# The odd rows of the first output chunk, stored by nine of the sixteen DMA engines over SP's and GpSimd's queues

## The reference, cut to what matters

```python
def _attn_ref(q, k, v, g_norm):                    # (8, 8, 576, 64) each
    kv = np.einsum('bhsd,bhse->bhde', k, v)
    out = np.einsum('bhsd,bhde->bhse', q, kv)
    rms = np.sqrt(np.mean(out * out, axis=-1, keepdims=True) + 1e-06)
    return out / rms * g_norm

def _moe_ref(x, phi, w1, w2):                      # x (4608, 512), phi (512, 32), 8 experts, 1024 hidden
    logits = x @ phi
    d = exp(logits - logits.max(0)); d /= d.sum(0) + 1e-09
    slot_input = (d.T @ x).reshape(8, 4, 512)
    for e in range(8):
        slot_out[e] = np.maximum(slot_input[e] @ w1[e], 0.0) @ w2[e]
    c = exp(logits - logits.max(1)); c /= c.sum(1) + 1e-09
    return c @ slot_out.reshape(32, 512)           # (4608, 512), float32
```

## Time and profile before

| | before |
|---|---|
| median of 3 runs | 172.56 us |
| the profiled execution's own time | 172.53 us |
| its span, first to last instruction | 171.2 us |
| mean share of time in which the 16 DMA engines were busy | 98.2% (three kinds of queue together) |
| moved | 71.67 MB, 419 GB/s over the span |
| PE / DVE / ACT / POOL busy | 149.1 / 86.0 / 88.9 / 57.2 us |
| issue of the four stores, SP | 144.24, 151.57, 157.04, 161.19 us |
| last store, issue to landing | 9.9 us |

### The profile page before, as it was taken

The page is one execution under the profiler, slowest core; times in us unless marked ns, Lnnn a source line. Parts: engine busy times, 40 slices in busy tenths (PEclk is TensorE's granted clock), DMA queues, the critical chain, the costliest instruction groups (busy, mean ns, idle before and its releaser), DMA issues.

```text
span 171.2 us, 4497 instructions
## 1 busy us (share of the span) xinstructions
PE 149.1 (87%) x1975; PEld 108.1 (63%) x1975; DVE 86.0 (50%) x184; ACT 88.9 (52%) x230; POOL 57.2 (33%) x68
## 2 busy tenths in 40 slices
PE   7787897989999899999899999999999988989400
PEld 3467776979688888898797775455565444445100
DVE  1122156283677265763936798724897027137400
ACT  2037576786965887768849864203213025137400
POOL 6000708548356755466482579200000000000000
PEclk9999999999999999999999999999999999999965
DMA  5999999999999999999999999998999999999995
GB/s 192 416 422 433 439 415 437 472 421 474 417 413 458 430 426 430 406 404 452 433 492 419 431 429 389 434 450 354 436 478 387 461 390 421 439 396 439 406 459 241
DMA packets 3476, 71.67 MB, mean 419 GB/s; under 512 B 384, under 2 KB 384, under 8 KB 384
## 3 DMA queue, kind: packets, MB, share of 16 engines
q1 hardware_dynamic: 3456, 71.38, 97.6%
HBM read 61.94 MB, written 9.44 MB: 417 GB/s over the span
## 4 chain that ended last, share of the span: by engine, by line
PE 47%; DMA 26%; ACT 12%; DVE 5%; SPq 2%; issue 1%
PE psum L204 47%; DMA arena<-in_kv_dram 13%; DMA arena<-in_w_dram 13%; ACT bd L204 3%; ACT sq L204 3%; ACT xall L204 2%; SPq L204 2%; DVE logits L204 1%; ACT arena L204 1%; DVE ms L204 1%; ACT part L204 1%; ACT d L204 1%; ACT r L204 1%; DVE r L204 0%; DVE d L204 0%
## 5 line engine op out<-in xcount | busy, mean ns | idle before, releaser
L204 PE MATMUL psum<-bd,arena 128*128 128x192 f32 (+1 forms) x320 | 56.1, 335 | 1.9 <-ACT bd L204 1.5
L204 PEld LDWEIGHTS psum<-bd,arena 128*128 128x128 f32 (+1 forms) x320 | 45.4, 179 | 7.1 <-ACT bd L204 2.8
L204 DVE TENSOR_REDUCE ms<-sq 128x16 f32<-128x1024 f32 (+1 forms) x19 | 22.1, 1162 | 32.6 <-ACT sq L204 32.3
L204 POOL TENSOR_TENSOR xall<-xall,r 128x512 f32<-128x512 f32 x34 | 34.8, 1044 | 0.0
L204 POOL TENSOR_TENSOR part<-part,r 128x512 f32<-128x512 f32 x17 | 17.8, 1049 | 49.7 <-DVE r L204 49.7
L204 ACT ACTIVATE sq<-psum 128x512 f32<-128x512 f32 x36 | 21.5, 598 | 12.6 <-PE psum L204 12.4
L204 PE MATMUL psum<-arena 128*64 128x64 f32 (+1 forms) x640 | 21.7, 226 | 3.3 <-DMA arena<-in_kv_dram 2.2
L204 PEld LDWEIGHTS psum<-arena 128*64 128x64 f32 (+1 forms) x640 | 19.0, 137 | 7.9 <-DMA arena<-in_kv_dram 3.5
L204 ACT COPY xall<-psum 128x512 f32<-128x512 f32 x34 | 20.6, 606 | 0.0
L204 ACT COPY part<-psum 128x256 f32<-128x256 f32 (+1 forms) x38 | 13.6, 359 | 9.9 <-DVE part L204 8.8
L204 DVE TENSOR_REDUCE logits<-part 128x64 f32<-128x512 f32 (+1 forms) x18 | 17.8, 991 | 0.0
(11 more groups left out here) (74 smaller groups left out, 118.9 us busy)
## 6 DMA issues: line engine op xcount, KB each, us to landing
arena<-in_w_dram SPq DMA_DIRECT2D x4, 4096.0 KB, 19.9
arena<-in_w_dram SPq DMA_DIRECT2D x1, 7168.0 KB, 27.5
arena<-in_t_dram SPq DMA_DIRECT2D x1, 6912.0 KB, 36.1
arena<-in_w_dram SPq DMA_DIRECT2D x1, 5120.0 KB, 17.9
arena<-in_kv_dram SPq DMA_DIRECT2D x2, 2304.0 KB, 23.4
arena<-in_kv_dram SPq DMA_DIRECT2D x1, 4608.0 KB, 42.6
out_dram<-arena SPq DMA_DIRECT2D x2, 2304.0 KB, 9.6
arena<-in_kv_dram SPq DMA_DIRECT2D x1, 3584.0 KB, 32.2
```

Source lines behind the costliest of these rows:

```text
L204: inst = getattr(engine, method)(*args, **kwargs)
```

## The change

The first store (chunks 0 to 2, 128 rows of 18432 bytes) is taken apart. The odd rows of chunk 0 (64 rows of 6144 bytes) are stored by themselves as soon as chunk 0 is there, in four transfers (`APART`): GpSimd's queue (POOL) stores 21 of them in a transfer whose outer dimension has 3 steps, and then 11 of them, each cut in two, with an outer dimension of 2; SP's queue stores 30 with an outer dimension of 5, and the last 2. When chunk 2 is there, SP stores the 64 even rows of all three chunks (18432 bytes each) and the 64 odd rows of chunks 1 and 2 (12288 bytes each). Two tiny transfers on GpSimd's queue (`step_over`, 7 and 5 rows of two pieces of 16 bytes, from an input into a scratch tile) stand ahead of the two stores of that queue. By the change's description the odd rows of chunk 0 are stored by DMA engines 0 to 4, 7 to 9 and 15 alone. The other three stores, all loads and all arithmetic stay as they are; the bytes are placed in the output in another order, and the host puts them back.

```diff
+CHUNK = 4 * 12 * 32
+APART = (("gpsimd", 11, 21, 3, 1), ("gpsimd", 0, 11, 2, 2), ("sync", 32, 30, 5, 1), ("sync", 62, 2, 2, 1))
+STEPS = (7, 5)
...
+    steps = const.tile([P, 16], F32, name="steps")
...
+    def step_over(n):
+        ends = [x[:n, : 2 * w].rearrange("p (c n) -> p c n", c=2)[:, :, :4] for x, w in ((steps, 8), (first_in, 64))]
+        nc.gpsimd.dma_start(*ends)
+
+    def store_apart():
+        at = 0
+        for j, (engine, lo, n, a, c) in enumerate(APART):
+            src = place(OUT_AT[0], CHUNK)[2 * lo + 1 : 2 * (lo + n) : 2]
+            size = n * CHUNK
+            dst = out[:, at : at + size].rearrange("o (b a n) -> (o a) b n", a=a, n=CHUNK // c)
+            if c > 1:
+                src = src.rearrange("p (c n) -> p c n", c=c)
+            getattr(nc, engine).dma_start(dst, src)
+            at += size
+            if j == 0:
+                step_over(STEPS[1])
+
+    def store_first():
+        at = 64 * CHUNK
+        for i in range(2):
+            n = (3 - i) * CHUNK
+            nc.sync.dma_start(out[:, at : at + 64 * n].rearrange("o (m n) -> (o m) n", n=n), place(OUT_AT[i], n)[i::2])
+            at += 64 * n
...
-        for row in OUT_ROWS:
+        if n == 0:
+            store_apart()
+        if n == 2:
+            store_first()
+        for row in OUT_ROWS[1:]:
...
+    step_over(STEPS[0])
     expert_h(0)
```

More of the change, by code:

```diff
@@ L262, in row_length, with apart_pieces @@
     return sum(UNIT if part is None else UNIT // 2 for _, _, part in row)
+def apart_pieces():
+    return [
+        np.array([(2 * m + 1, h, c) for m in range(lo, lo + n) for h in range(c)]).reshape(a, -1, 3).swapaxes(0, 1).reshape(-1, 3)
+        for _, lo, n, a, c in APART
+    ]
 def soft_moe_linear_attention(nc, first_in, kv_in, q0_in, q1_in, kv4_in, kv5_in, t3_in, w_in, out):
@@ L1029 @@
     n = 4 * CT * NS
-    chunks = []
-    for row in OUT_ROWS:
+    three = np.empty((P, 3 * n), np.float32)
+    at = 0
+    for pieces in apart_pieces():
+        for p, h, c in pieces:
+            w = n // c
+            three[p, h * w : h * w + w] = res[0, at : at + w]
+            at += w
+    three[::2] = res[0, at : at + 192 * n].reshape(64, 3 * n)
+    three[1::2, n:] = res[0, at + 192 * n : 3 * P * n].reshape(64, 2 * n)
+    chunks = [three[:, k * n : k * n + n] for k in range(3)]
+    for row in OUT_ROWS[1:]:
         part = res[0, row[0] * n * P : (row[-1] + 1) * n * P].reshape(P, len(row), n)
```

## The result

| | before | after |
|---|---|---|
| median | 172.53 us (172.40 to 172.65, 6 runs) | 173.18 us (173.02 to 173.26, 6 runs) |
| ratio after / before | | 1.0037, 95% interval 1.0024 to 1.005 |
| the profiled execution, its span | 172.53, 171.2 | 173.15, 171.8 |
| issue of the last three stores | 151.57, 157.04, 161.19 | 151.83, 157.31, 161.45 |

The change is slower by 0.65 us. The forecast was 171.75, and 173.18 lies outside its range.

The account below looks back on a forecast made before the run. DMA engines working off stores were taken to bound the end. Moving it from 170.6 to 169.8 gains 0.8 us, other costs nothing: 172.53 - 0.8 = 171.73, plus 0.03 for the median, so 171.75 us; range 171.4 to 173.0.

Parts of the forecast that it names:

- What bounds the kernel: At the program's end: DMA engines working off stores set the end, the last store landing at 171.1 of 171.2 us.
- If the seven spared engines are the seven late ones, each of them ends 0.91 us sooner.: Last store: engines 5, 6, 10 to 14 lose four odd rows each and end at 169.6 to 169.8.
- The latest of the nine between 169.3 and 170.1, I take 169.8.: Last store: end of the nine early engines, which get 2, 3 or 7 more rows; total gain 0.8 us.
- the idle time: Around the second and last stores' issues: 5.8 engine-us on early engines, to take up most of 6.4 engine-us of added rows.
- GpSimd's transfers: nothing.: GpSimd's queue at 108 and chunk 0: its issues and packets cost nothing, coming long before 151.57.
- SP's issues, and every other row: SP's added issues at chunks 0 and 2, 0.33 to 0.35 us each, cost nothing; reading alternate rows was left to a rival.
- Rival 2: Stores of every other row: two engines may share a part of SBUF; priced at +2 us, 173.8 us; chance 0.12.
- A store issue later than 161.2: Last store's issue: a sign that the forecast is wrong, with loads delayed and PE's wait before 144.49 longer.
- Rival 1: The engine with eleven rows isn't early and ends last: 172.9 us, or 174.1 if among the seven late; chance 0.08.
- Rival 4: Late and spared engines agree only in part, or one with three more rows is late: 172.5 us; chance 0.08.

Follow-up runs that it names:

- no11_step6: The change without GpSimd's eleven-row store, SP storing 16 rows over 16 engines, 25 in five parts, 2 in two, plus a tiny 6-row GpSimd transfer; median 173.49 us, profiled 171.86.
- sp_only: The change without GpSimd's queue: SP stores 32 odd rows over all 16 engines, 30 in five parts, 2 in two; median 172.25 us, ratio 0.9995.
- gp_only: The change with GpSimd's rows as they are and SP's 32 odd rows spread over all 16 engines; 172.57 us, ratio 1.0008.
- split16: The first store split as in the change, but all 64 odd rows in one SP transfer over 16 engines, nothing on GpSimd's queue; 172.58 us, ratio 0.9997.
- e_before: The kernel before with sixteen tiny marker loads between the last load and the first store of SP's queue, to tell engines apart; 173.89 us.

## Why the prediction was wrong

- **What bounds the kernel.** Right: the DMA engines working off stores set the end.
- **"If the seven spared engines are the seven late ones, each of them ends 0.91 us sooner."** Right in kind. 5, 6 and 10 to 14 are the late ones of the kernel before, and thirteen engines of the profile after land by 170.64. Where nothing else came in the way the gain was exact (no11_step6: 170.35 for 170.38). sp_only's 170.67 for 170.60 is in part luck, since its last engine is another one.
- **"The latest of the nine between 169.3 and 170.1, I take 169.8."** This is the step that failed. Its upper bound took an engine with three rows more and no idle time, but one of the early nine of the profiled execution. I had written that "the windows don't name engines" and still bounded the nine by where they stood in one execution. A late engine with two or three rows more lands at 171.06 + 0.46 to 0.68 = 171.52 to 171.74. The last engine of the profile after is such a one, with two rows more, at 171.67, and the eleven-row engine follows at 171.33. Nor did the idle time cover the nine: in the kernel before five of them have 0.85 to 1.45 us each and the other four at most 0.26. The term should have had the late engine as its upper end, a loss of 0.7 us. The forecast, a gain of 0.8, missed by 1.4.
- **"GpSimd's transfers: nothing."** Too low: 352 small packets on all engines, 0.2 us an engine, so that the late engines of gp_only gained 0.3 us of 0.46. The first packet comes 3.5 us after the issue, which cost nothing, as said.
- **SP's issues, and every other row.** Right, nothing (split16), though two of the sizes were off: SP's issues at chunks 0 and 2 took 0.52 to 0.95 us and not 0.33 to 0.35, in time that was free, and no packet of 3072 bytes exists, since all of GpSimd's 32 rows move as packets of 6144. Rival 2, with 0.12, was wrong, and with it the rule of "Door 1" in the Trainium skill's "SBUF — State Buffer" made no difference here. Engines 7 and 15 aren't slower than the rest either, as "Latency and other measured facts" in "DMA: Bandwidth & Descriptors" would have it: both are among the first in e_before, 145.99 and 146.32.
- **"A store issue later than 161.2" as a sign.** It came, 161.45, behind loads that were later by 0.26 us, which is within what this landing scatters by; it touches only engines that wait for the issue.
- **Rival 1** had the right kind of mechanism, an engine with extra rows that isn't early, and its two prices, 172.9 and 174.1, stand around the 173.18. It was tied to the eleven-row engine alone and had 0.08. **Rival 4** named what happened, an engine with more rows that "is itself among the late", but priced it at 172.5 and also gave it 0.08; 172.53 + 0.46 to 0.68 would have made it 173.0 to 173.2. With nine engines, of which one late is enough, the two together deserved a multiple of their 0.16.

## What to carry to other kernels

A transfer cut unevenly over DMA engines is a bet on which engines are behind; before it is made, the landings of several executions should show that the same ones always are. Where they are put back by instruction fetches, an even kernel is steady and an uneven one gains 0.7 us in one execution and loses 1.0 in the next. Expect of small transfers on GpSimd's queue that they put packets on all 16 engines. No version here beats the kernel before with certainty; the nearest is sp_only, 172.25 in the median but 0.9 to 1.3 us above its fastest run in three of eleven.

## What the runs showed that was not expected

- One instruction fetch of 16384 bytes takes 0.88 to 0.97 us of one DMA engine and sets it back by more than that; at 141.42, after 14 of them, the engines are spread over 3.0 us.
- The packet right behind a fetch is slow too: 0.4 us over its usual time (18432 bytes at 151.28 before, 12288 at 152.99 after).
- GpSimd's queue starts its first packet 3.5 to 4.0 us after the issue (142.50 to 146.02; 108.12 to 112.1), and its 21-row store takes 9.2 us to land where SP's 64-row store takes 8.8.

```profile
out_dram<-arena SPq DMA_DIRECT2D x1, 1152.0 KB, 8.8
...
out_dram<-arena POOLq DMA_DIRECT2D x1, 126.0 KB, 9.2
out_dram<-arena POOLq DMA_DIRECT2D x1, 66.0 KB, 11.8
```
